# First expert weights loaded one head earlier in one burst, and the clearing of two scratch tensors moved from ScalarE's queue to SyncE's, in an attention plus mixture-of-experts kernel

## The reference

```python
q_bits = (np.einsum('bhsd,dk->bhsk', q, proj) > 0)     # and k_bits
mask = q_bucket[:, :, :, None] == k_bucket[:, :, None, :]
scores = np.where(mask, scale * q @ k.T, -1e9)
attn = exp(scores - rowmax) / sum
x = attn @ v                                            # 1536 rows of 512
```

## Time and profile before

| what | before |
|---|---|
| median of three runs | 831.32 us |
| the profiled execution: its time, its span | 831.7 us, 829.6 us |
| granted TensorE clock, mean | 0.971 |
| TensorE matmul busy | 91% |
| VectorE, ScalarE, GpSimd busy | 54%, 43%, 28% |
| bytes moved by DMA | 92.24 MB |

### The profile page before, as it was taken

One profiled execution on the slowest core, in us unless ns is written; L12 is line 12 of the kernel. 1 busy time (PEld: TensorE's weight loads), 2 busy tenths in 40 slices (PEclk: granted clock), 3 DMA queues, 4 the chain that ended last, 5 costly groups with the idle time before them and its releaser, 6 DMA issues.

```text
span 829.6 us, 11762 instructions
## 1 busy us (share of the span) xinstructions
PE 756.4 (91%) x4117; PEld 618.5 (75%) x4117; DVE 445.5 (54%) x698; ACT 358.1 (43%) x543; POOL 232.3 (28%) x237
## 2 busy tenths in 40 slices
PE   3899999999999995089999999949999999999998
PEld 2677777777777763079999999938888888888886
DVE  4668777877777678345555666514344222322221
ACT  2454556555555553045555566514333322332223
POOL 3157676576767674501111010100000000000000
PEclk9999999999999998579999999979999999999999
DMA  5674444454544302447656665444001100010001
GB/s 120 180 195 119 115 109 120 126 144 119 131 117 116 90 1 107 158 166 248 209 206 210 231 225 176 177 160 161 1 1 51 51 1 1 0 52 1 1 0 51
DMA packets 62735, 92.24 MB, mean 111 GB/s; under 512 B 29935, under 2 KB 31983, under 8 KB 62192
## 3 DMA queue, kind: packets, MB, share of 16 engines
q1 hardware_dynamic: 54416, 76.05, 30.4%
q10 hardware_dynamic: 6048, 9.48, 3.5%
q0 software_dynamic: 2240, 6.30, 2.0%
HBM read 58.76 MB, written 19.94 MB: 95 GB/s over the span
## 4 chain that ended last, share of the span: by engine, by line
PE 81%; ACT 6%; DVE 5%; DMA 3%; issue 3%; POOL 2%; SPq 0%; POOLq 0%; ACTq 0%; DVEq 0%
PE score_ps L1355 11%; PE score_ps L1357 11%; PE score_ps L1356 11%; PE out_pair L1357 7%; PE out_pair L1355 7%; PE out_pair L1356 7%; PE score_ps L1194 3%; ACT probs L711 3%; PE out_pair L1249 3%; PE out_pair L1251 3%; PE out_pair L1250 3%; PE out_pair L1264 2%; PE score_ps L1223 2%; PE prep_ps L1180 2%; PE score_ps L1231 2%
## 5 line engine op out<-in xcount | busy, mean ns | idle before, releaser
L605 POOL TENSOR_TENSOR probs_lo<-probs,probs_hi 128x768 fp32r<-128x768 f32 x62 | 113.5, 1851 | 102.2 <-ACT probs_hi L715 101.9
L1355 PE MATMUL score_ps<-w_hi,h_hi 128*128 128x512 f32 x320 | 126.3, 395 | 0.4 <-DVE h_lo L1143 0.4
L1357 PE MATMUL score_ps<-w_hi,h_lo 128*128 128x512 f32 x320 | 124.7, 390 | 0.0
L1356 PE MATMUL score_ps<-w_lo,h_hi 128*128 128x512 f32 x320 | 124.6, 389 | 0.0
L1355 PE MATMUL out_pair<-xT_hi,w_hi 128*128 128x512 f32 (+1 forms) x320 | 112.2, 351 | 0.0
L1136 DVE SCALAR_TENSOR_TENSOR gated<-tclip,out_pair 128x512 f32<-128x512 f32 x48 | 33.0, 688 | 145.2 <-ACT tclip L838 145.2
L1357 PE MATMUL out_pair<-xT_hi,w_lo 128*128 128x512 f32 (+1 forms) x320 | 110.9, 346 | 0.0
L1356 PE MATMUL out_pair<-xT_lo,w_hi 128*128 128x512 f32 (+1 forms) x320 | 110.9, 346 | 0.0
L914 DVE TENSOR_REDUCE rowmax<-score_ps 128x1 f32<-128x768 f32 x96 | 88.7, 952 | 19.3 <-PE score_ps L1194 18.9
L838 ACT ACTIVATE tclip<-out_pair,three 128x512 f32<-128x512 f32 x48 | 33.2, 692 | 146.3 <-PE out_pair L1357 146.3
L1081 DVE TENSOR_TENSOR w_lo<-w_raw,w_hi 128x1024 fp32r<-128x1024 f32 x72 | 85.9, 1223 | 18.6 <-ACT w_hi L725 18.3
(11 more groups left out here) (150 smaller groups left out, 1300.3 us busy)
## 6 DMA issues: line engine op xcount, KB each, us to landing
w_raw<-in_moe_w SPq DMA_DIRECT2D x32, 1024.0 KB, 7.1
x_slots<-zrow ACTq DMA_DIRECT2D x12, 513.0 KB, 4.1
rows_in<-x_slots SPq DMA_DIRECT2D x8, 513.0 KB, 8.6
w_raw<-in_moe_w_in SPq DMA_DIRECT2D x4, 1024.0 KB, 6.8
w_raw<-in_moe_w_out SPq DMA_DIRECT2D x4, 1024.0 KB, 13.6
qk_raw<-in_q SPq DMA_DIRECT2D x16, 192.0 KB, 3.3
qk_raw<-in_k SPq DMA_DIRECT2D x16, 192.0 KB, 3.4
v_raw<-in_v SPq DMA_DIRECT2D x16, 192.0 KB, 2.4
```

The source lines that it names most:

```text
L605: g.tensor_tensor(probs_lo[:, kc, :], probs[:, kc, :], probs_hi[:, kc, :].bitcast(F32), ALU.subtract).then_inc(lo_done_p, 1)
L1355: mm(out_tile, lhs[0], rhs[0], start=first, stop=False)
L1356: mm(out_tile, lhs[0], rhs[1], start=False, stop=False)
L1357: return mm(out_tile, lhs[1], rhs[0], start=False, stop=last)
```

## The change

SyncE issues all four loads of the first expert's weights in one run, after `place_head` of head 0 and before `next_head` of head 1. ScalarE and GpSimd do their pieces of that split one head earlier: ScalarE in heads 1, 3, ... 13 (and one before the last head, as before), GpSimd in heads 2, 4, ... 14 (and one after the last head, as before). Because ScalarE waits for all four loads ahead of its first piece, that wait now stands before its head 1 and not before its head 2. The scratch tensors are cleared in 6 pieces in place of 12, twice as large (1026 KB and 512 KB), and SyncE issues them, one piece in each turn of its loop: after `load_v` that ends `next_head` of an odd head 2 * turn + 1, and ahead of `next_head` of head 2 * turn + 2.

```diff
-    CLEARS = HEADS - 4
+    CLEARS = HEADS // 2 - 2
@@ SyncE
             place_head(Head(0, 0), first=True)
+            for s in range(LOADS):
+                load_part(0, s, of_expert(0, s), raw_in[s])
-            def next_head(h, between=None):
+            def next_head(h):
                 load_qk(h.next())
                 place_head(h)
-                if between:
-                    between()
                 load_v(h.next())
-            def first_weights(half):
-                for s in range(half * LOADS // 2, (half + 1) * LOADS // 2):
-                    load_part(0, s, of_expert(0, s), raw_in[s])
-            next_head(Head(0, 1), between=lambda: first_weights(0))
-            next_head(Head(1, 0), between=lambda: first_weights(1))
+            def clear_piece(n):
+                sp.dma_start(slots_pieces[n, :, :, :], ...).then_inc(zero_out, 16)
+                sp.dma_start(rows_pieces[n, :, :, :], ...).then_inc(zero_out, 16)
+            next_head(Head(0, 1))
+            next_head(Head(1, 0))
+            sp.wait_ge(zrow_set, 1)
             with sp.Fori(1, HEADS // 2 - 1) as turn:
-                for h in (Head(turn, 1), Head(turn + 1, 0)):
-                    next_head(h)
+                next_head(Head(turn, 1))
+                clear_piece(turn - 1)
+                next_head(Head(turn + 1, 0))
@@ GpSimd
-            head(Head(1, 0))
+            head(Head(1, 0), spare=lambda: first_low(0))
             with pool.Fori(1, HEADS // 2 - 1) as turn:
-                head(Head(turn, 1), spare=lambda: first_low(turn - 1))
-                head(Head(turn + 1, 0))
-            head(LAST, last=True, spare=lambda: first_low(CHUNKS - 2))
+                head(Head(turn, 1))
+                head(Head(turn + 1, 0), spare=lambda: first_low(turn))
+            head(LAST, last=True)
@@ ScalarE
             head(first, first=True)
-            head(first.next())
             for s in range(LOADS):
                 act.wait_ge(raw_in[s], 16)
-            act.wait_ge(zrow_set, 1)
-            with act.Fori(1, HEADS // 2 - 1) as turn:
-                head(Head(turn, 0), spare=lambda: high_parts(0, turn - 1))
-                clear_piece(turn * 2 - 2)
-                head(Head(turn, 1))
-                clear_piece(turn * 2 - 1)
-            head(LAST.prev(), spare=lambda: high_parts(0, CHUNKS - 2))
+            with act.Fori(0, HEADS // 2 - 1) as turn:
+                head(Head(turn, 1), spare=lambda: high_parts(0, turn))
+                head(Head(turn + 1, 0))
             high_parts(0, CHUNKS - 1)
```

More of the change, by code:

```diff
@@ L418, in _ @@
             place_head(Head(0, 0), first=True)
-            def next_head(h, between=None):
+            for s in range(LOADS):
+                load_part(0, s, of_expert(0, s), raw_in[s])
+            def next_head(h):
                 load_qk(h.next())
                 place_head(h)
-                if between:
-                    between()
                 load_v(h.next())
-            def first_weights(half):
-                for s in range(half * LOADS // 2, (half + 1) * LOADS // 2):
-                    load_part(0, s, of_expert(0, s), raw_in[s])
-            next_head(Head(0, 1), between=lambda: first_weights(0))
-            next_head(Head(1, 0), between=lambda: first_weights(1))
+            slots_pieces = x_slots.rearrange("(n r p) c -> n p r c", p=P, n=CLEARS)
+            rows_pieces = y_rows.rearrange("(n r p) c -> n p r c", p=P, n=CLEARS)
+            def clear_piece(n):
+                sp.dma_start(slots_pieces[n, :, :, :],
+                             zrow[:, :].unsqueeze(1).to_broadcast([P, SLOTS // P // CLEARS, XC])).then_inc(zero_out, 16)
+                sp.dma_start(rows_pieces[n, :, :, :],
+                             zrow[:, 0:DM].unsqueeze(1).to_broadcast([P, NT // CLEARS, DM])).then_inc(zero_out, 16)
+            next_head(Head(0, 1))
+            next_head(Head(1, 0))
+            sp.wait_ge(zrow_set, 1)
             with sp.Fori(1, HEADS // 2 - 1) as turn:
-                for h in (Head(turn, 1), Head(turn + 1, 0)):
-                    next_head(h)
+                next_head(Head(turn, 1))
+                clear_piece(turn - 1)
+                next_head(Head(turn + 1, 0))
             place_head(LAST)
@@ L743, in head @@
                     exps(h, c, first)
[L745 to L752, removed]
             first = Head(0, 0)
```

## The result

The change made the kernel 5.4% slower: 876.33 us (median of four runs, 875.14 to 880.29) against 831.51 us, a ratio of 1.0545 with a 95% interval of 1.051 to 1.0581. Timed again beside the experiments it took 869.9 us against 831.51 (ratio 1.0439, 1.0402 to 1.0476). The forecast was 838.5 us, range 834.6 to 843. The profiled execution is quicker than all four of these: 867.35 us, span 865.4 us, 35.8 us longer than before. All that follows on places is from that execution, so some 9 us of the median's loss are not in it.

What follows compares the result with a forecast made beforehand. TensorE, busy 91% of the span, was taken as the bound, so only what makes it wait counts. The late bits of head 1 add 7.2 us, all else 0: 831.3 + 7.2 = 838.5 us, range 834.6 to 843.

Steps and rivals of the forecast that it cites:

- The burst: Start: four weight loads queued ahead of head 1's moves delay its bits from 25.36 to 32.6 us, +7.2 us (+4.4 to +9.4).
- Four issues, then q and k, SyncE is free again at 18.3: Start: issues from 14.76 us take 2.3 plus 1.2 us, so SyncE is free before ScalarE releases the move at 20.50.
- ScalarE's new wait costs nothing: After head 0's exponentials: the four loads end by 28.4 us, the exponentials after 40, so the wait costs nothing.
- Weight pieces earlier: Loop: ScalarE's and GpSimd's weight pieces one head earlier fall into waits or idle gaps; cost 0.
- ScalarE's freed issues: Loop: 24 clear issues of about 0.4 us leave ScalarE, 9.6 us in all; taken as 0 (rival "Faster", 0.04: 826.5 us).
- Clears on SyncE's queue: Loop: piece behind v's load takes 4.3 us at 364 GB/s, 0.9 us left before the moves' data is due; cost 0.
- the prediction's upper bound: Clears in the loop: piece at 248 GB/s takes 6.3 us, moves 1.1 us late, 6.6 us in six turns.
- The rival: Loop: clears on SyncE's queue hold the moves up too, 6 x 1.1 us on top, 845.1 us; chance 0.12.
- The price of a late move: Loop, in the clears rival: 1.1 us late per turn costs 6.6 us in six turns; clock effect weighed only at the start.
- Nearly no slack: Loop: head's moves have almost no margin; the second lands at 80.12 us and the bits start at 80.22.

Runs made afterwards that it cites:

- the weights alone: Changed kernel with the clears put back to 12 single pieces on ScalarE's queue, weight burst and earlier weight pieces kept: 838.09 us against 830.38, ratio 1.0092.
- the filler control: Kernel before the change plus 20 small TensorE matmuls ahead of the late wait in heads 1, 3, ... 13: 869.9 us against 830.65, ratio 1.0451.

## Why the prediction was wrong

- *The burst*: right in mechanism and place, and in size within what repeats differ by. Bits at 32.69 against 32.6, 7.7 us when run alone against 7.2; in the profile with the weights alone they came at 33.53, so the agreement to 0.1 us is luck.
- *"Four issues, then q and k, SyncE is free again at 18.3"*: wrong, it was held until 23.9, without an effect that the traces show.
- *ScalarE's new wait costs nothing*: right for this change, but only because the burst stood so early; the run with the burst behind head 1 shows what it costs otherwise.
- *Weight pieces earlier, ScalarE's freed issues*: both 0, as forecast.
- *Clears on SyncE's queue*: this is the step that failed. It let the piece of 1.57 MB run at the 364 GB/s of a half-size piece for 4.3 us and found 0.9 us to spare. The piece started at that rate and then fell to 53 to 96 GB/s for 3 us; it took some 7.2 us, more also than the 6.3 us of the prediction's upper bound. A half-size piece ends before that lasts; its tail in the earlier trace rows (248 GB/s over the longer stretch) was the hint, and was read as a mean rate and not as a piece that slows after its first part. The rival had the mechanism (clears hold the moves up) at 1.1 us a turn; the bits waited 2.7 us on the mean ((26.2 - 7.2 - 2.6) / 6).
- *The price of a late move*: the second thing that was missing. The rival passed a late move on one for one, 6.6 us in six turns; the loop lost 29.1 us, 10.4 of idle TensorE and 18.7 of TensorE at a lower granted clock. The prediction had weighed the clock for the start alone and took 0 there. "Nearly no slack" was wrong the other way: a wait of the bits of 0.93 us cost 0.04 us.
- The sum of the rival, 845.1 us, was thus short by 31 us, and the range ended below it.

## What to carry to other kernels

A transfer of twice the size can take more than twice the time: before doubling one that stands ahead of short, urgent copies, read its last microsecond, not its mean rate, and ask when the engines are free again. When a TensorE that hardly ever waits is made to wait in every turn of a loop, price the wait and then the slower matmuls after it; here the second was nearly twice the first. A burst of loads that nobody waits for soon can still hold up the small copies queued behind it.

## What the runs showed of the hardware

- A clear of 1.57 MB into HBM reached 376 to 394 GB/s in its first 2 us, then ran at 39 to 127 GB/s for 2 to 3 us with the DMA engines shown busy (0.78 to 1.41), then at 156 to 387 GB/s again, on either queue and at two places in a head. Four loads of 1 MB from HBM in one run showed no such stretch once they flowed (311 to 410 GB/s in each microsecond from 17 to 28 us).
- With four loads of 1 MB issued, SyncE's next issues took 2.5 and 3.7 us in place of 0.6.
- TensorE's granted clock fell in each of the six heads with a late move of the changed kernel. With q and k ahead of the piece it fell in the three heads with a wait of 1.54 to 1.56 us and in none of the two with 0.99 us. In the filler control it fell in four of seven heads, each with an idle time of 1.05 us and 20 small matmuls behind it.
